# Transposes of the identity into a free PSUM bank, in TensorE's queue of the first unit

## The reference

```
for t in range(S):                       # B, H, S, D = 4, 8, 768, 48
    cur = einsum('bhd,bhe->bhde', u * k[t], v[t])
    y[t] = einsum('bhd,bhde->bhe', r[t], state + cur)
    state = w[t][..., None] * state + einsum('bhd,bhe->bhde', k[t], v[t])
x = y as rows of (B * S, H * D)          # 3072 x 384
h = x @ w_in                             # 3072 x 1024
solu = h * softmax(h)
x = (solu - mean) / sqrt(var + 1e-6) * g_ln @ w_out
x = relu(x @ moe2_w_in) ** 2 @ moe2_w_out    # 384 -> 2048 -> 384
```

## Time and profile before

| | |
|---|---|
| median of 3 runs | 794.96 us (793.18 to 801.43) |
| profiled execution | 795.18 us |
| its span, first to last instruction | 793.5 us |
| TensorE matmul busy | 749.8 us (95%) |
| TensorE weight load busy | 634.6 us (80%) |
| VectorE busy | 494.6 us (62%) |
| ScalarE busy | 445.3 us (56%) |
| GpSimd busy | 158.0 us (20%) |

### The profile page before, as it was taken

The page is one execution under the profiler, slowest core; times in us unless marked ns, Lnnn a source line. Parts: engine busy times, 40 slices in busy tenths (PEclk is TensorE's granted clock), DMA queues, the critical chain, the costliest instruction groups (busy, mean ns, idle before and its releaser), DMA issues.

```text
span 793.5 us, 25802 instructions
## 1 busy us (share of the span) xinstructions
PE 749.8 (95%) x10624; PEld 634.6 (80%) x10624; DVE 494.6 (62%) x1075; ACT 445.3 (56%) x967; POOL 158.0 (20%) x242
## 2 busy tenths in 40 slices
PE   2669989999999999999999999999999999999997
PEld 2549778778897888888788888788888788888886
DVE  6795986866658657647747646755746852543333
ACT  5786875765656736644745645664664672433322
POOL 5342240231321312211312120321320310000000
PEclk9988999999999999999999999999999999999999
DMA  6606725945543560632542543534354333344652
GB/s 177 216 23 196 257 71 198 331 185 198 192 147 121 194 220 34 241 138 89 201 163 90 179 161 127 200 112 143 103 193 146 120 121 126 119 159 143 212 192 91
DMA packets 34021, 125.54 MB, mean 158 GB/s; under 512 B 5104, under 2 KB 10608, under 8 KB 33904
## 3 DMA queue, kind: packets, MB, share of 16 engines
q1 hardware_dynamic: 33264, 123.13, 44.4%
q10 hardware_dynamic: 640, 0.75, 0.4%
HBM read 105.39 MB, written 17.30 MB: 155 GB/s over the span
## 4 chain that ended last, share of the span: by engine, by line
PE 81%; DMA 6%; DVE 5%; ACT 4%; issue 3%; SPq 2%; DVEq 0%; ACTq 0%
PE hid L667 24%; PE acc L684 23%; PE flex L648 11%; PE flex L617 10%; PE flex L547 4%; PE flex L631 3%; DMA w<-split_w 2%; PE flex L587 2%; PE flex L574 2%; PE flex L562 1%; ACT att L1056 1%; ACT r_right L1056 1%; PE flex L598 1%; SPq L405 1%; DVE r_t L839 1%
## 5 line engine op out<-in xcount | busy, mean ns | idle before, releaser
L667 PE MATMUL hid<-y_hi,w 128*128 128x512 f32 (+1 forms) x624 | 202.6, 382 | 1.6 <-DMA w<-split_w 0.8
L684 PE MATMUL acc<-g_hi,w 128*128 128x512 f32 (+1 forms) x624 | 199.9, 380 | 1.9 <-DVE g_lo L928 1.3
L1291 POOL TENSOR_TENSOR k_t<-k_t,w_up 128x256 f32<-128x256 f32 x120 | 86.2, 734 | 296.0 <-PE flex L547 253.6
L924 DVE TENSOR_TENSOR act<-act 128x512 f32<-128x512 f32 (+1 forms) x104 | 70.0, 673 | 113.4 <-ACT g_hi L1056 113.2
L667 PEld LDWEIGHTS hid<-y_hi,w 128*128 128x128 f32 x624 | 115.0, 188 | 25.2 <-DMA w<-split_w 2.2
L684 PEld LDWEIGHTS acc<-g_hi,w 128*128 128x128 f32 x624 | 114.9, 188 | 24.3 <-issue 2.1
L1056 ACT ACTIVATE r_right<-r_t 64x256 f32<-64x256 f32 x240 | 100.1, 417 | 34.9 <-DVE r_t L839 31.8
L667 PE MATMUL hid<-y_lo,w 128*128 128x512 f32 (+1 forms) x312 | 116.7, 374 | 0.0
L684 PE MATMUL acc<-g_lo,w 128*128 128x512 f32 (+1 forms) x312 | 116.7, 374 | 0.0
L1056 ACT ACTIVATE act<-hid 128x512 f32<-128x512 f32 (+1 forms) x104 | 58.6, 564 | 97.7 <-PE hid L667 97.2
L648 PE MATMUL flex<-ln_hi,out_hi 128*128 128x256 f32 x288 | 81.6, 283 | 0.0
(11 more groups left out here) (114 smaller groups left out, 1200.3 us busy)
## 6 DMA issues: line engine op xcount, KB each, us to landing
w<-split_w SPq DMA_DIRECT2D x88, 768.0 KB, 4.5
split_w<-w SPq DMA_DIRECT2D x16, 768.0 KB, 6.0
r_t<-in_rT SPq DMA_DIRECT2D x11, 512.0 KB, 6.7
w_t<-in_wT SPq DMA_DIRECT2D x11, 512.0 KB, 5.2
k_t<-in_kT SPq DMA_DIRECT2D x11, 512.0 KB, 6.4
v_n<-in_vN SPq DMA_DIRECT2D x12, 384.0 KB, 3.9
out<-o_stage SPq DMA_DIRECT2D x5, 768.0 KB, 4.3
o_stage<-in_w2in SPq DMA_DIRECT2D x16, 192.0 KB, 3.7
```

The costliest lines, as they stand in the source:

```text
L667: last = mm(hid[:, cols], w2[:, step % RING, w, k * P:(k + 1) * P], y[:, k, cols], start=n == 0, stop=n == len(terms) - 1)
L684: last = mm(acc[:, d, cols], w2[:, step % RING, w, rows], gx[:, step % 2, cols], start=j == 0 and n == 0, stop=j == final and n == 2, skip ...
L924: e.tensor_tensor(act[:, step % 2, cols], act[:, step % 2, cols], act[:, step % 2, cols], ALU.mult).then_inc(g_ready, 1)
L1291: e.tensor_tensor(halves(k_t[K_BUF[l + 1]][:, half(h)], l)[:, :, 0, :], left, right_w, ALU.mult).then_inc(k_ready[h], 1)
```

## The change

A helper `keep_busy(u, n)` puts n transposes of the identity into `flex` bank 2, columns 0 to 127, in the first unit alone. It is called behind each half of `k_natural` (4 each), behind `output` (5) and behind `state_step` (6): nineteen instructions in all. They wait for nothing and raise nothing; nobody reads what they write, and the first product of `hidden1` writes the bank anew. The other engines' queues are the same.

```diff
--- before.py
+++ after.py
@@ -552,6 +552,12 @@
                                   right[:, :, o // 2:o // 2 + BK], start=True, stop=True)
                 last.then_inc(level_mm[h], 1)
 
+            def keep_busy(u, n):
+
+                if u == 0:
+                    for _ in range(n):
+                        nc.tensor.transpose(flex[:, MLP1, 0:P], ident[:, :], ident[:, :])
+
             def k_natural(u):
 
                 for h in range(2):
@@ -561,6 +567,7 @@
                         x = HX * h + n
                         last = nc.tensor.transpose(flex[:, h, n * P:(n + 1) * P], k_t[K_BUF[LEVELS]][:, x * P:(x + 1) * P], ident[:, :])
                     last.then_inc(knat_mm, 1)
+                    keep_busy(u, 4)
 
             def read_state(u):
 
@@ -587,6 +594,7 @@
                         last = mm(flex[head_rows(out_half(u, i, b2)), b2, x * T:(x + 1) * T], v_n[rows, x % NBH, head_cols(x, i)],
                                   att[rows, x, i], start=not u and x == 0, stop=x == NX - 1, skip_group_check=True)
                 last.then_inc(y_mm, 1)
+                keep_busy(u, 5)
 
             def state_step(u):
 
@@ -598,6 +606,7 @@
                         last = mm(flex[head_rows(i), b2, x * D:(x + 1) * D], k_nat[rows, x, head_rows(i)],
                                   v_n[rows, x % NBH, head_cols(x, i)], start=True, stop=True)
                 last.then_inc(state_mm, 1)
+                keep_busy(u, 6)
 
             def hidden1(u, t, f):
```

## The result

The changed kernel takes 802.5 us (median of 20 runs, 799.85 to 808.37), the kernel before 795.83 us (20 runs, 791.31 to 801.43). The ratio is 1.0087, 95% interval 1.0071 to 1.0103: slower by 6.7 us. The profiled execution took 803.93 us, with a span of 802.2 where before had 793.5.

What follows compares the result with a forecast made beforehand. Prediction: TensorE's own queue bounds the kernel behind the start, a VectorE, transfer and ScalarE chain before it. 795.18 + 0 (cost) - 0 to 0.05 (gain) = 795.15, on the median's scale 794.9 us; range 791.8 to 798.2.

Steps and rivals of the forecast that it cites:

- What bounds the kernel: From about 100 us on, TensorE's own full queue; in the first unit, a chain through VectorE, small transfers and ScalarE.
- no case here reaches 1% alone: Claim that neither the forecast nor any rival by itself changes the time by 1%, 8 us.
- Cost of the added work: First unit: nineteen transposes, 4.2 us of TensorE, fit into its pauses; 0 to 0.2 us on the path, taken as 0.
- The two pauses called just full: Behind output products (five transposes) and state products (six): the first just full, the second 0.03 us over.
- Gain from the clock: First unit: earlier rise to 2.4 GHz saves at most 2.2 us of TensorE; 0 to 0.05 us arrives.
- the new wait for r_right: Ahead of the second unit's level 1: TensorE, done with nine products sooner, waits; level 1 still starts at 41.2 us.
- The row: Trace sign: the clock came back at 64.4 us after transposes alone from 59.6 us, so transposes can raise it.
- The rule of the Trainium skill: TensorE transposes don't count as busy in the same way for the clock gate; the rise would stay at about 40 us.
- The first rival: First unit: the clock's rise stays at about 40 us; price 0 to 0.2 us, 794.9 to 795.1 us; chance 0.18.
- the second: Start of the kernel: the clock's gain gets through, 2.2 us, or 4.7 with the second stretch; 790.2 to 792.7; chance 0.13.
- The third: Clock falls in the new pause before 41.2 us, slowing 27 products by 5.7 us; 797.9 to 800.6; chance 0.07.
- The second stretch at the lower clock: Second unit, 54.2 to 64.4 us: TensorE at 1.2 GHz, forecast to stay unchanged; 2.5 us less if its transposes ran fast.

Runs made afterwards that it cites:

- e5: Changed kernel plus 218 cheap instructions (78 waits at the start, 35 small products ahead of level 3), 256 added in all: 794.71 us, ratio 1.0006.
- e1: Changed kernel with its nineteen transposes replaced, at the same four places, by 38 waits on a semaphore raised long before: 801.41 us, ratio 1.0074.
- e2: Changed kernel plus 218 waits on a long-raised semaphore in the first unit, 150 of them ahead of TensorE's first work: 802.9 us, ratio 1.0088.
- e8: Changed kernel plus 218 instructions, mostly 2-column products, in the tenth unit's state step at about 536 us: 800.36 us, ratio 1.0069.

## Why the prediction was wrong

The prediction was 794.9 us, 791.8 to 798.2; measured 802.5.

**What bounds the kernel.** The step that failed is the first: "behind the start the time is TensorE's own queue, and the change adds nothing there". It adds nothing to the queue but moves the queue's blocks. The page of before had the hint, an "instruction" queue and the word "issue" as a releaser, and I priced neither. Hence no rival named it, and "no case here reaches 1% alone" rested on cases of the first 66 us only.

**Cost of the added work: 0 on the path.** Right for the first unit: the added transposes fitted, the state products started at 32.25 where 31.97 was worked out, and e5 shows the whole change at no cost once the borders are back. The two pauses called just full took their transposes without making anything late: output and state products came 0.28 and 0.29 us late against the earlier trace rows, but so did the first transposes of k, ahead of all that was added. The missing term is 38 instructions of shift, 6.7 us by the medians: two gaps (1.92 and 2.97 us) and a spell of lower clock behind each.

**Gain from the clock: 2.2 us of TensorE time, nobody waits for it.** Right. The rise came at 28.8 us, just ahead of the forecast 29 to 37, the nine products took 1.6 us less, and level 1 began where it did, now with the new wait for r_right that was forecast. e5, with the early rise, equals the kernel before.

**Transposes and the clock.** The row was the right guide: with transposes in the pauses the clock rose at 28.8 and 29.4 us, with waits in the same places at 38.6 us (e1). The rule of the Trainium skill quoted in the prediction ("TensorE: Matmul & The Clock Gate", Part 4: PE-mode transpose) doesn't hold for the transposes of this kernel; whether they run in the mode that the page means, no trace says.

**The first rival** (nothing happens to the clock) didn't occur, **the second** (the gain gets through) neither. **The third** did occur: the clock fell at 42.5 us behind the new pause, and about eight of the 27 products were slow, short of the ten from which the prediction let it decide. It cost 1.7 us on TensorE instead of 5.7, and e5, in which it fell at 43.0 us too, shows that none of it arrives. The second stretch at the lower clock was forecast unchanged; it lay from 56.1 to 63.0 us instead of 54.2 to 64.4.

A page that would have helped: the Trainium skill, "Runtime: NRT & Kernel Launch", Instruction fetch mechanics, says that a program is fetched in blocks of 16 KiB, 256 instructions, the next one while the current one runs, and that crossing a border is mostly hidden. The trace agrees on the size (16.4 KB, 85 packets) and on the order; that it is hidden doesn't hold here at the 35 borders with a gap, where TensorE came to the border sooner than 2.2 to 2.8 us after the load had started.

## What to carry to other kernels

An instruction that is added to an engine with a long straight program moves every later block border of that engine. Where bursts of small products run through 256 instructions in two or three microseconds, compare the same change with its instruction count filled up to a whole block before believing that the work or the order made the difference. Two gaps of 2 to 3 us with "issue" as their releaser, in a series that needs nothing new, are the sign to look for.

## What the runs showed of the hardware

- From going over a border to running the next block took 4.2 us with idle transfer engines (556.6 to 560.75), and 5.3 us behind a transfer of weights (655.45 to 660.73). From the start of the block's load to running it took 2.2 to 2.8 us at all 35 gaps.
- Shifts of 38, 80 and 128 instructions cost 0.7 to 0.9%, 1.8% and 2.2% of this kernel; 232 cost 0.3% and 256 nothing that can be measured.
- A gap of TensorE of 2 to 3 us cost 1.4 to 1.6 us more, since the granted clock was 1.2 GHz for a spell behind it (0.50 in the windows at 562 and 661 us). With the gap of 1.4 us at 561 us in e1 the granted clock stayed at 2.4 GHz.
- Waits on a semaphore long since raised took 106 ns of TensorE's queue each (150 of them from 1.0 to 17.1 us in e2).
- Products of 2 columns into one spot took 40 ns a matmul in e8, 32 ns until the clock fell at 537.0 us and 53 ns after. It fell while TensorE was busy with them, from 534.75 us on.
